# The first expert block in two parts: 384 rows listed before the attention has ended, 256 rows from the complete routing

## What is computed

```python
attn = softmax(scale * q @ k.T + bias)          # 32 heads of 576 x 576
x = (attn @ v) as 2304 tokens x 512
noisy = x @ w_gate + log1p(exp(x @ w_noise)) * noise
top2, weights = the two largest of 8, softmax of the two
for e in range(8):                              # E
    rows = tokens with e in top2
    out[rows] += weight * (relu(x[rows] @ w1[e]) @ w2[e])   # 512 -> 1024 -> 512
```

## Time and profile before

| | |
|---|---|
| median of three runs | 834.14 us (831.83 to 835.36) |
| the profiled execution | 833.52 us, of which its span is 831.6 us |
| PE busy | 769.2 us, 92% |
| DVE, ACT, POOL busy | 496.7, 388.6, 379.1 us |

### The profile page before, as it was taken

The page is one execution under the profiler, slowest core; times in us unless marked ns, Lnnn a source line. Parts: engine busy times, 40 slices in busy tenths (PEclk is TensorE's granted clock), DMA queues, the critical chain, the costliest instruction groups (busy, mean ns, idle before and its releaser), DMA issues.

```text
span 831.6 us, 18549 instructions
## 1 busy us (share of the span) xinstructions
PE 769.2 (92%) x6642; PEld 622.8 (75%) x6642; DVE 496.7 (60%) x1208; ACT 388.6 (47%) x828; POOL 379.1 (46%) x435
## 2 busy tenths in 40 slices
PE   4886999999999994399999999999999999999994
PEld 2345766776776762298898898998998998988983
DVE  5997898998999967854435335336335344353310
ACT  5995888887887865023224224233233232241200
POOL 0017998998998950541342333324324414412212
PEclk9996999999999997599999999999999999999998
DMA  7785344443443453270571542623704805714023
GB/s 167 210 229 128 109 121 112 126 131 100 135 137 93 126 183 123 65 267 16 83 234 33 127 171 50 170 108 65 236 27 76 253 2 84 244 13 51 2 26 38
DMA packets 51175, 97.17 MB, mean 117 GB/s; under 512 B 12640, under 2 KB 21472, under 8 KB 51104
## 3 DMA queue, kind: packets, MB, share of 16 engines
q1 hardware_dynamic: 39920, 74.55, 29.5%
q0 software_dynamic: 10320, 21.41, 14.1%
q10 hardware_dynamic: 864, 0.29, 0.2%
HBM read 65.07 MB, written 20.53 MB: 103 GB/s over the span
## 4 chain that ended last, share of the span: by engine, by line
PE 83%; DMA 5%; DVE 4%; ACT 4%; issue 2%; POOL 1%; ACTq 0%; SPq 0%; POOLq 0%; DVEq 0%
PE ps L768 27%; PE po L783 24%; PE po L655 11%; PE ps L575 8%; PE pt L602 6%; DMA out_rows<-ys,iscat 2%; PE pt L581 2%; DMA slab<-work 2%; ACT work L1131 2%; ACT work L1112 2%; PE pt L616 1%; PE pt L589 1%; DVE ohlo L1017 1%; DMA qraw<-in_qT 1%; DMA work<-in_pcol 1%
## 5 line engine op out<-in xcount | busy, mean ns | idle before, releaser
L768 PE MATMUL ps<-xT,whi 128*128 128x320 f32 x1024 | 176.1, 309 | 0.9 <-ACT xT L1233 0.9
L1244 ACT ACTIVATE hT<-ps 128x320 fp32r<-128x320 f32 x128 | 55.9, 437 | 231.8 <-PE ps L768 212.3
L783 PE MATMUL po<-whi,hT 128*128 128x512 f32 x640 | 162.5, 398 | 0.0
L768 PEld LDWEIGHTS ps<-xT,whi 128*128 128x128 f32 x1024 | 156.2, 187 | 1.7 <-issue 1.1
L1064 DVE SCALAR_TENSOR_TENSOR hT<-ps,hT 128x320 fp32r<-128x320 f32 x128 | 62.7, 491 | 153.0 <-ACT hT L1244 133.3
L783 PEld LDWEIGHTS po<-whi,hT 128*128 128x128 f32 x640 | 118.1, 188 | 26.9
L1350 POOL DMA_INDIRECT out_rows<-ys,iscat x40 | 68.5, 1712 | 133.6 <-DMA out_rows<-ys,iscat 74.7
L1299 POOL TENSOR_SCALAR work<-work,rcp 128x576 f32<-128x576 f32 (+1 forms) x160 | 117.7, 745 | 24.0 <-DVE rcp L862 23.2
L1147 ACT ACTIVATE work<-ns,nmax 128x576 f32<-128x576 f32 (+1 forms) x160 | 123.1, 769 | 4.1 <-DVE nmax L849 4.1
L849 DVE CUSTOM_DVE_ANT_0 ns<-ps,slab 128x576 f32<-128x576 f32 (+1 forms) x160 | 119.9, 750 | 8.2 <-PE ps L575 4.3
L1337 POOL DMA_INDIRECT xg<-x_rows,igath x30 | 32.4, 1080 | 152.0 <-DVE ys L1079 78.5
(11 more groups left out here) (140 smaller groups left out, 1091.7 us busy)
## 6 DMA issues: line engine op xcount, KB each, us to landing
wraw<-in_mw SPq DMA_DIRECT2D x64, 512.0 KB, 7.2
slab<-work SPq DMA_DIRECT2D x36, 288.0 KB, 3.8
qraw<-in_qT SPq DMA_DIRECT2D x64, 144.0 KB, 2.9
vs<-in_v SPq DMA_DIRECT2D x32, 160.0 KB, 2.4
out_rows<-zeros SPq DMA_DIRECT2D x32, 152.0 KB
kraw<-in_kT SPq DMA_DIRECT2D x64, 72.0 KB, 2.5
x_rows<-xnat SPq DMA_DIRECT2D x8, 576.0 KB, 4.2
wrow<-w_rows,iscat POOLq DMA_INDIRECT x40
```

The lines of the kernel that those rows point to most:

```text
L768: mm = nc.tensor.matmul(bank, w1s[i][pw][:, c, f * P:(f + 1) * P], xT[px][:, c, half * HB:(half + 1) * HB], start=j == 0 and c == 0, stop= ...
L783: mm = nc.tensor.matmul(po[:, (i + t) % 2, :], hT[px][:, c, t * P:(t + 1) * P], w2s[i][pw][:, c, :], start=j == 0 and c == 0, stop=j == 2 ...
```

## The change

Expert 0's block is no longer run whole in the loop. Its first 384 rows (`HA`, three tiles) are taken from the tokens of the first twelve list tiles, which belong to the first three images, and its other 256 rows from the complete routing.

- In the attention, at tile 135 (`FOLD`) and after it: the logits of these tokens, their noise, maxima and indices, and the mask of expert 0 (`early_routing`, `softplus`).
- In the drain: two small matmuls that count (`rank0_ready`), positions, 12 one-hot matrices on VectorE, 12 matmuls that make three columns of the list (`list0_ready`), three row lists, and three gathers (`routed0`). SP loads expert 0's W1 during head 30 and its W2 soon after; ScalarE and VectorE split W1 between their other work.
- After the last head: TensorE transposes the three tiles and does the first layer of the 384 rows, its first four groups pass by pass with the low part of W1 last, then the counts of the complete routing, then groups 4 to 7 and the second layer. VectorE writes the low parts of `hT` between the steps of the complete routing. The low parts of W2 are made on GpSimd instead of VectorE.
- Beside the second layer of this part, the two lists are made; then come 256 rows with eight groups of 12 matmuls with 256 columns, and two tiles of the second layer. The positions of the complete routing count expert 0 as having at least 384 rows so far (`short`).
- The one-hot matrices now carry the token number (a second scalar), so that `rhsa` and the second step of `rhsb` are gone. The loop runs blocks 1 and 2, 3 and 4, 5 and 6, and block 7 is behind it.
- The bias table is stored head first, which frees the space of the first heads for W1; the memory of the expert phase is laid out anew.

```diff
+HA = XB * P
-NLA, NLB = BT, NL - BT
+NLA, NLB = BT - XB, NL - BT
+FOLD = GLAG + (H - 1) * NU + (B - 2) * H * NU + 2
+NEARLY = 2 * CL
@@ sync
+                if n == B * H - 2:
+                    sp.wait_ge(ttr_done, (B * H - 5) * NU)
+                    load_expert(0, 0, range(W1C))
+            sp.wait_ge(ttr_done, (B * H - 3) * NU)
+            load_expert(0, 0, range(W1C, NC))
@@ tensor, drain and first part
+            pe.wait_ge(oh0_done, NEARLY + 1)
+            lists(NEARLY, ohlo, oh0, ps[1][:, 1, 0:XB]).then_inc(list0_ready, 1)
             pv(B * H - 1, range(NU))
...
+            xa = [xTa[px][:, :, :] for px in range(2)]
+            for j, (px, pw) in enumerate(((0, 0), (1, 0), (0, 1))):
+                if j == 1:
+                    pe.wait_ge(xlo_done, C_XLO + XB)
+                if j == 2:
+                    pe.wait_ge(w_split, W1C)
+                for f in range(4):
...
+                    first(0, f, f, j, px, pw, xa, HA)
+            pe.wait_ge(x_done, NX)
+            pe.wait_ge(r_rank, 1)
+            flat = both[:, :, :].rearrange("p t e -> p (t e)")
+            nc.tensor.matmul(pt[0][:, 0:NT * NE], tri, flat, start=True, stop=True)
...
+            for f in range(4, CF):
+                if f % 2 == 0:
+                    pe.wait_ge(hlo_done, C_HLO + f - 2)
+                for j, (px, pw) in enumerate(PASSES):
+                    first(0, f, f, j, px, pw, xa, HA)
+
+            pe.wait_ge(w2_split, NC - W1C)
+            pe.wait_ge(hlo_done, C_HLO + CF)
+            for t in range(XB):
+                pe.wait_ge(y_done, C_Y + t - 1)
+                second(0, t)
+                if t == 1:
+                    pe.wait_ge(rhs_done, 1)
+                    pe.wait_ge(oh_done, 2 * NT)
+                    lists(2 * NT, ohlo, oha, pt[1][:, 0:NLA]).then_inc(lista_ready, 1)
+            pe.wait_ge(rhs_done, 2)
+            lists(2 * NT, ohlo, rhsb, pt[0][:, 0:NLB]).then_inc(listb_ready, 1)
@@ gpsimd
+            pool.wait_ge(routed0, 1)
+            for t in range(XB):
+                gather(igath[1][:, t:t + 1], t, (B - 1) * S)
+            for c in range(W1C, NC):
+                pool.wait_ge(w_hi, c + 1)
+                nc.gpsimd.tensor_tensor(wlo[0][:, c * WC:(c + 1) * WC], wraw[0][:, c * WC:(c + 1) * WC],
+                                        whi[0][:, c * WC:(c + 1) * WC].bitcast(F32), ALU.subtract).then_inc(w2_split, 1)
```

More of the change, by code:

```diff
@@ L303, in build @@
             rpad = tmp("rpad", [P, NL])
+            tmp("above", [P, (nc.sbuf_top - 2 * WE * 4 + CD * F * 4 - nc.sbuf_base) // 4])
+            xTa = [tmp(f"xTa{i}", [P, CD, HA], F32R) for i in range(2)]
             late.close()
@@ L780, in block_of @@
                     pe.sem_inc(pe_passed, 1)
-                    for j, (px, pw) in enumerate(PASSES):
-                        for c in range(CF):
-                            mm = nc.tensor.matmul(po[:, (i + t) % 2, :], hT[px][:, c, t * P:(t + 1) * P],
-                                                  w2s[i][pw][:, c, :],
-                                                  start=j == 0 and c == 0, stop=j == 2 and c == CF - 1)
-                    mm.then_inc(y_ready, 1)
+                    second(i, t)
@@ new lines, in after, with part, copied @@
+            def after(ins):
+                done[0] += 1
+                ins.then_inc(r_dve, 1)
+                dve.wait_ge(r_dve, done[0])
+            V = nc.vector
+            def part(ap, cs):
+                return ap[:, 2 * cs[0]:2 * cs[-1] + 2, :]
+            def copied(cs, half, src):
+                dve.wait_ge(lt_ready, half + 1)
+                V.tensor_copy(part(logit[:, :, :], cs).rearrange("p t e -> p (t e)"), src[:, 0:len(cs) * 32])\
+                    .then_inc(lt_copied, 1)
+                dve.wait_ge(lt_copied, half + 1)
@@ new lines, in perturbed @@
+            def perturbed(cs, half):
+                dve.wait_ge(r_act, 2 * half + 2)
+                pairs = "p (c a) e -> p c a e"
+                drawn = wnoise[:, :, :].rearrange("p (a c) e -> p c a e", a=2)[:, cs[0]:cs[-1] + 1, :, :]
+                after(V.tensor_tensor(part(noisy[:, :, :], cs).rearrange(pairs, a=2),
+                                      part(ez[:, :, :], cs).rearrange(pairs, a=2), drawn, ALU.mult))
+                after(V.tensor_tensor(part(noisy[:, :, :], cs), part(noisy[:, :, :], cs),
+                                      part(logit[:, :, 0:NE], cs), ALU.add))
@@ new lines, in xlow0, with hlow0 @@
+            def xlow0(t, src):
+                dve.wait_ge(xhi_done, t + 1)
+                cols = slice(t * P, (t + 1) * P)
+                V.tensor_tensor(xTa[1][:, :, cols], src.rearrange("p (c t) -> p c t", c=CD),
+                                xTa[0][:, :, cols].bitcast(F32), ALU.subtract).then_inc(xlo_done, 1)
+            def hlow0(n):
+                half, f = divmod(n, CF)
+                cols = slice(0, HA) if half == 0 else slice(HA, BLK)
+                dve.wait_ge(hhi_done, n + 1)
+                V.scalar_tensor_tensor(out=hT[1][:, f, cols], in0=ps[n % 4 // 2][:, n % 2, 0:cols.stop - cols.start], scalar=0.0,
+                                       in1=hT[0][:, f, cols].bitcast(F32), op0=ALU.max, op1=ALU.subtract)\
+                    .then_inc(hlo_done, 1)
@@ L939, in _ @@
+            after(V.tensor_tensor_scan(inc[:, 0, early], ones[:, early], tot[:, 0, early], 0.0, ALU.mult, ALU.add))
             evac0(TILES - 6)
             recip(TILES - 1)
-            evac0(TILES - 5)
-            copied(early, 0)
+            after(V.tensor_tensor(pre[:, 0, early], inc[:, 0, early], tot[:, 0, early], ALU.subtract))
+            after(V.tensor_tensor(pos[:, early, 0], ps[0][:, 0, early], pre[:, 0, early], ALU.add))
+            after(V.scalar_tensor_tensor(out=posk[:, early], in0=pos[:, early, 0], scalar=1.0, in1=both[:, early, 0],
+                                         op0=ALU.add, op1=ALU.mult))
@@ L943, in _ @@
+            one_hots([(i, 2 * i) for i in range(6)], oh0_done)
             evac0(TILES - 4)
-            perturbed(early, 0)
+            one_hots([(i, 2 * i) for i in range(6, NEARLY)], oh0_done)
+            V.tensor_scalar(short[:, :], inc[:, 0, NEARLY - 1:NEARLY], float(HA), float(-HA), ALU.min, ALU.add).then_inc(r_dve, 1)
+            done[0] += 1
             evac0(TILES - 3)
             evac0(TILES - 2)
-            indexed(early)
+            split(0, 0, 0, 0)
+            dve.wait_ge(list0_ready, 1)
@@ L1251, in block_of @@
                         xcopy(BT * (b + 1) + t, (i + 1 + t) % 2, t)
-            for g in range(XB):
-                xcopy(g, g % 2, g)
+            xcopy(3, 1, 3)
+            xcopy(4, 0, 4)
+            for n in range(CF, 2 * CF):
+                hhigh0(n)
+                if n % 2:
+                    split(1, W1C + n // 2 - CF // 2, 1)
+            for c in range(W1C):
+                split(1, c, 1)
+            xcopy(5, 1, 0)
+            xcopy(6, 0, 1)
+            xcopy(7, 1, 2)
             act.wait_ge(blocks_done, 1)
```

536 lines of the change are left out of this document (338 added, 198 removed).

## The result

The changed kernel took 821.75 us (median of four runs, 821.45 to 824.17) against 834.75 us (831.83 to 837.84) for the kernel before on the same chip: ratio 0.985, 95% interval 0.981 to 0.989. In a later session it took 824.75 us against 831.82, ratio 0.9907, 0.9883 to 0.9931. So it is faster by 0.9 to 1.5%, by 0.7 to 1.9% with the intervals. The profiled execution took 821.77 us.

The account below looks back on a forecast made before the run. PE bounds 83% of the chain, but from 319.8 to 354.3 us DVE's serial routing does. Block 1 20.3 us earlier, less attention 4.0, port 5.0, clock 2.3, gives 9.0: 833.5 - 9.0 = 824.5, 825 against the median; range 815 to 832.

Parts of the forecast that it names:

- block 1's start: First 320-column matmul, after block 0: forecast at about 403.7 us against 412.75 before.
- the likeliest case: Whole kernel: 825 us, chance 0.50, bounds 820.5 to 830 from attention 2 to 7, port 3 to 8, 256 columns up to 2.8.
- Prices on PE: First layer of block 0: matmuls of 384 columns cost 0.176 us, of 256 columns 0.118, possibly 0.147 if weight load set the pace.
- Attention and drain: Early routing in attention adds 4.0 us (1.5 matmuls, 2.5 DVE); in the drain, last product with V starts at 312.4, not 313.58.
- The port: Part one: POOL's four W2 subtractions hold short DVE instructions with SBUF input and output; 5 us taken, bounds 0 and 9.6.
- the 3 us that were to make the prediction wrong: Sign of failure: another wait, for W1's low part in the third pass or a gather under loads, longer than 3 us.
- the port holds nothing up: Rival, chance 0.27: POOL's subtractions in part one do not delay DVE, group 7's wait stays 3.7 us; 818 us.
- The one-hots: DVE in part one, ahead of the eighth low part: eighteen one-hots take 2.9 us; above 0.165 each the prediction is wrong.
- The lists: PE beside part one's second layer: short list 2.4 us and long list 2.5 us.
- The clock in the wait: PE's wait from 339.0 to 347.7 us brings the clock down; 4.6 us of work at half speed cost 2.3.
- The clock in part one: Rival, chance 0.06: gather waits halve the clock, part one's first-layer matmuls take 33.8 us instead of 16.9; 842 us.
- The change leaves blocks 1 to 7 as they are: Behind block 0 the dense stream stays unchanged, so only block 1's start was forecast.

Follow-up runs that it names:

- second profile: The changed kernel, unedited, measured and profiled once more beside the variants of Experiment 6: 824.75 us, ratio 0.9907.
- Experiment 6: Changed kernel with W2's four low parts for expert 0 subtracted on VectorE instead of GpSimd: 822.54 us, against 824.75 for the unedited changed kernel beside it.
- experiment 4: Kernel before with a second scalar operand, a column of ones, multiplied in its 36 one-hots: 835.93 us, ratio 1.001.
- experiments 5 and 8: Changed kernel with 38 unread matmuls behind group 7: 823.69 us; changed kernel with hT's low parts 5 to 7 moved ahead of the one-hots: 820.25 us.
- Experiments 1 and 2: Kernel before with the changed kernel's expert-phase SBUF layout: 829.27 us; with only 960 unused bytes ahead of hT: 829.56; with only hT ahead of xT: 832.26.
- experiment 9: Changed kernel with hT's low parts ahead of the one-hots, W2's low parts on VectorE, and one-hots with one scalar: 821.97 us, ratio 0.9845.

## Why the prediction was right, and where it was not

The time (825, range 815 to 832) was right, and so was the mechanism: the dead 34 us became a wait behind group 7 for the eighth low part. The forecast for block 1's start, 403.7, was met at 404.62, but by a sum of errors and in part by luck. On a count from 209 us the gain there is 5.6 (4.4 in the second profile), not 9.0. The upper end of the likeliest case, 830, doesn't follow from its own bounds: attention 7, port 8 and 2.8 for the 256 columns together make 834.

- **Prices on PE.** Right. 384 columns: eight in 1.39 us, 0.174 (0.176 said). 256 columns: four in 0.455 us at full clock, 0.114 (0.118 said), and not the bound of 0.147.
- **Attention and drain.** The last `qk` went from 300.22 to 301.98 with a start 2.54 us ahead: 4.3 us, where 4.0 were said. The last product with V came 3.6 us later on that count, against the 2.8 of "312.4 rather than 313.58" and the 4.0. The first 384-column matmul came at 324.62, 327.2 on that count, where 325 was said.
- **The port.** The mechanism was right and the term undersized: 7.9 us of hold (2.2 + 1.5 + 2.1 + 2.1) against the 5 taken, inside the bounds of 0 and 9.6 (7.0 in the second profile). Experiment 6 shows the cause. That the hold would also reach PE, at W1's last low part, was not in the sum: 1.90 us, below the 3 us that were to make the prediction wrong, and hidden on PE's side behind VectorE's longer queue. What DVE could do beside POOL's subtractions, maxima and reads from PSUM, filled much less than the "half of that time" that the text assumed. The rival that the port holds nothing up (0.27) was wrong.
- **The one-hots.** "18 one-hots 2.9" failed: they took 4.2 us. The text had named 0.165 each as what would make it wrong; experiment 4 shows that the second scalar with its multiplication is the cause.
- **The lists.** Oversized: 2.4 and 2.5 us said, by a row at half clock; at full clock they took 0.9 and 1.5. This gave back 2.5 us of what the other terms cost more.
- **The clock in the wait.** Right in kind, 2.3 said. By the eight matmuls in 3.55 instead of 1.83 us it cost 1.7.
- **The clock in part one.** The rival that gave it 0.06 had it at half through the whole first layer. In four of eight profiles it was at half for 3 to 4 us, in part one or around its start; in the profiled execution this made sixteen matmuls 1.5 us longer.
- **The clock ahead of part two** was missing from the sum. The first layer of part two ran at 0.50 from 378 to 381 after waits of about a microsecond each, which cost some 1.5 us. What experiments 5 and 8 lost on the way went mostly into the waits themselves (1.0 and 1.8 us more than in the profile after) and less into part two's slower start (0.4 and 1.1). The waits are for part two's rows: their gathers landed 6.2 to 7.4 us after they were issued (profile after), the first of them beside loads of weights at some 400 GB/s, where rows 6 and 7 have 3.4 us. That the loads are the cause was not tested.
- **"The change leaves blocks 1 to 7 as they are"** failed. The new layout made the 512-column matmuls faster, 3.6 us behind block 1's start. Experiments 1 and 2 show this: 960 bytes of offset, in a line of the diff that looks like bookkeeping. It made good much of what the terms above cost more than said, which was luck: without it, and without the head start at 209 us, the profiled execution would have taken about 833.5 - 5.6 = 827.9 us against the forecast of 824.5.

## What to carry to other kernels

When a dead stretch is filled, look at the one queue that now feeds the waiting engine, and ask of every instruction in it ahead of the awaited one whether anyone needs it so soon; here 18 one-hots stood ahead of a low part without need. Work that is given to GpSimd holds a VectorE instruction with two inputs in SBUF until it ends (7.0 and 7.9 us of 9.7 and 9.5 in two profiles), and the reverse holds for gathers that GpSimd begins beside a long tensor_tensor. And when a change moves buffers, measure the layout alone, or its effect is booked to the idea.

## What the runs showed of the hardware

- The place of the stationary operand's buffer in SBUF bears on the pace of matmuls: 512 columns against `hT` 0.233 us apart; with `hT` 960 bytes further up 0.226 in block 0 and 0.227 to 0.229 in later blocks; 0.229 in the changed kernel. Why the last ones differ is open.
- A second [P, 1] scalar operand, with the multiplication that uses it, in a tensor_scalar of 128x128 in 16 bits costs 0.06 us: 0.165 to 0.225.
- VectorE instructions with two inputs in SBUF (tensor_tensor of 128x1 to 128x1024, a scan of 128x144) that began beside one of GpSimd's subtractions were held until it ended; maxima, and instructions with an input in PSUM, ran beside it at their usual length (six maxima in 0.51 us).
- Two or three waits of 0.7 to 2.1 us close together, ahead of part two, were followed by 3 to 7 us at half clock in the changed kernel and in every variant of it. Behind the wait of 3.16 us in experiment 9 the clock stayed at 1.00, behind its next one, of 3.15 us, it fell to 0.50. After a wait of 1.9 us in part one it fell in one profile of the changed kernel and not in the other. So the length of one wait doesn't decide it in these rows.
- Eight executions of the changed kernel and its variants, whose edits all come later, stood up to 2.8 us apart at 209 us (the unedited kernel's two 1.7 us), so single profiles are to be compared from a common position, not from their start.
